# A further wait for GpSimd in the first group of a feed-forward stage, on one Trainium2 core

## The reference

```
x = attention(r, k, v, w, u)            # 4 x 768 tokens, 8 heads of 48: 3072 x 384
h = x @ w_in                            # 384 -> 2048
g = h - tanh(h)
x2 = g @ w_out                          # 2048 -> 384
e = argmax(normalised(x2) @ normalised(expert_emb).T / tau)
out = gate * (relu(x2 @ w1[e]) @ w2[e]) # 384 -> 1024 -> 384
```

## Time and profile before

| what | value |
|---|---|
| median of 3 runs | 871.93 us (870.47 to 874.06) |
| the profiled execution | 876.53 us, its span 874.8 us |
| busy: TensorE, VectorE, ScalarE, GpSimd | 845.3, 566.1, 482.6, 283.6 us |
| mean granted clock of TensorE | 0.981 of full speed |
| first group, masked copy of step 0 to that of step 15 | 128.93 to 199.58 us |

### The profile page before, as it was taken

The page is one execution under the profiler, slowest core; times in us unless marked ns, Lnnn a source line. Parts: engine busy times, 40 slices in busy tenths (PEclk is TensorE's granted clock), DMA queues, the critical chain, the costliest instruction groups (busy, mean ns, idle before and its releaser), DMA issues. The chain is left out here.

```text
span 874.8 us, 19145 instructions
## 1 busy us (share of the span) xinstructions
PE 845.3 (97%) x5568; PEld 742.6 (85%) x5569; DVE 566.1 (65%) x887; ACT 482.6 (55%) x1074; POOL 283.6 (32%) x321
## 2 busy tenths in 40 slices
PE   7999989999999999999999999999999999999995
PEld 6767758788998998998998998889899899989984
DVE  7979949999999999999999997512111211111120
ACT  4657766568777777877867866033332332333231
POOL 4434525323333433433343332212222232222211
PEclk8989999999999999999999999799999999999998
DMA  8999942215877877877877887298876576611100
GB/s 210 294 271 257 261 145 80 73 55 173 287 230 248 283 241 234 287 241 227 307 227 237 272 308 226 80 344 313 313 277 212 202 250 218 226 33 48 42 2 1
DMA packets 99370, 180.01 MB, mean 206 GB/s; under 512 B 10219, under 2 KB 25725, under 8 KB 99328
## 3 DMA queue, kind: packets, MB, share of 16 engines
q1 hardware_dynamic: 92000, 163.87, 57.8%
q0 software_dynamic: 3968, 10.82, 3.7%
q10 hardware_dynamic: 3360, 4.79, 1.7%
HBM read 114.96 MB, written 65.86 MB: 207 GB/s over the span
## 5 line engine op out<-in xcount | busy, mean ns | idle before, releaser
L1162 POOL TENSOR_TENSOR ew_l<-ew_raw,ew_h 128x512 fp32r<-128x512 f32 x96 | 126.5, 1325 | 215.0 <-DVE poly L1380 210.7
L1077 PE MATMUL y_ps<-wout_h,g_h 128*128 128x392 f32 x384 | 132.0, 344 | 3.0 <-ACT x_sb L1281 2.6
L1078 PE MATMUL y_ps<-wout_l,g_h 128*128 128x392 f32 x384 | 130.5, 340 | 0.0
L1079 PE MATMUL y_ps<-wout_h,g_l 128*128 128x392 f32 x384 | 130.4, 340 | 0.0
L1534 DVE TENSOR_TENSOR ex_hT_l<-e_bank,ex_hT_h 128x512 fp32r<-128x512 f32 x62 | 40.0, 686 | 125.3 <-ACT ex_hT_h L1690 125.3
L1077 PE MATMUL h_ps<-xT_h,win 128*128 (+1 forms) x288 | 114.4, 397 | 5.9 <-DVE diff L1361 5.0
L1079 PE MATMUL h_ps<-xT_h,win 128*128 (+1 forms) x288 | 113.9, 395 | 0.0
L1078 PE MATMUL h_ps<-xT_l,win 128*128 (+1 forms) x288 | 113.3, 393 | 0.0
L1261 ACT ACTIVATE g_h<-poly 128x512 fp32r<-128x512 f32 x96 | 61.0, 636 | 86.8 <-DVE poly L1380 86.1
L1690 ACT ACTIVATE ex_hT_h<-e_bank 128x512 fp32r<-128x512 f32 x62 | 33.8, 597 | 120.2 <-PE e_bank L1604 116.2
L1569 POOL DMA_INDIRECT out_dram<-ex_o_sb,put_i x31 | 31.1, 1002 | 205.2 <-ACT ex_o_sb L1674 205.2
(11 more groups left out here) (188 smaller groups left out, 1842.1 us busy)
## 6 DMA issues: line engine op xcount, KB each, us to landing
ew_raw<-in_w SPq DMA_DIRECT2D x96, 256.0 KB, 3.5
w_h<-ew_h SPq DMA_DIRECT2D x96, 256.0 KB, 3.6
w_l<-ew_l SPq DMA_DIRECT2D x96, 256.0 KB, 2.9
w_ex<-w_h SPq DMA_DIRECT2D x14, 1536.0 KB, 11.5
w_ex<-w_l SPq DMA_DIRECT2D x14, 1536.0 KB, 15.4
kv_sb<-in_kv SPq DMA_DIRECT2D x24, 384.0 KB, 7.4
krT_sb<-in_krT SPq DMA_DIRECT2D x40, 192.0 KB, 7.2
x_dram<-xt_sb ACTq DMA_DIRECT2D x48, 96.0 KB, 5.7
```

The costliest lines, as they stand in the source:

```text
L1077: pe.matmul(out, lh, rh, start=start, stop=False)
L1078: pe.matmul(out, lh, rl, start=False, stop=False)
L1079: return pe.matmul(out, ll, rh, start=False, stop=stop)
L1162: pool.tensor_tensor(ew_l[:, slot, :], raw, ew_h[:, slot, :].bitcast(F32), ALU.subtract).then_inc(ew_l_made, 1)
```

## The change

In `group` of GpSimd's program the condition `not is_first(g)` goes away, so that group 0 waits for `g_done` too, once a step, before the step's first piece. Everything else is as it was; on every engine the instructions stand in the order in which they stood.

```diff
                     for f in range(KF):
                         if last and f == KF - 1:
                             pool.wait_ge(gl_done, KF * CH)
-                        elif not is_first(g):
+                        else:
                             wait_apart(pool, passed_pool, (g_done, KF * g + f + 1))
                         for j in pieces_at(g, last, f):
                             low(g, j)
```

## The result

The changed kernel takes 861.63 us (median of 4 runs, 861.34 to 865.28) against 872.65 us before (median of 4). The ratio on record is 0.9886, with a 95% interval of 0.9851 to 0.992; it is not the plain quotient of the two medians, which is 0.9874. The same kernel in a second series took 864.75 us against 872.5, with a ratio of 0.9925 (0.9897 to 0.9953). It is faster, by about 1%; how much of the 11 us of the first series belongs to the change is what the experiments had to settle. The steps with one piece came out as long as forecast and those with two 0.18 us shorter, and VectorE gained 8.3 us where 6.83 were forecast.

The account below looks back on a forecast made before the run. VectorE was taken to bound steps 1 to 8 of the first group, about level with TensorE in the rest. Gains 0.64 + 4.75 + 1.44 = 6.83 us off 871.93 gave 865.1 us, range 861.8 to 869.0.

Parts of the forecast that it names:

- The start: First group, VectorE's line 1376 before the first masked copy: that copy comes 0.64 us earlier.
- Single pieces: First group from step 8, one GpSimd piece a step: four g_l shorter by 0.36 us each, 1.44 us less.
- Pairs: First group, eight intervals with two GpSimd pieces a step: 40.19 us becomes 35.44, 4.75 us less.
- 1.12 + 1.99 + 1.32: Two-piece interval of 4.43 us: masked copy to GpSimd's start, the pair's length, the pair's end to the next copy.
- the profiled run's 4.6 us: Whole kernel: the profiled execution lies 4.6 us above the median, and this difference was taken to carry over.
- What was costed at nothing: Behind the new wait: SyncE's raw-slot refills, TensorE's reads of win's low halves, the second group's stores; all cost nothing.
- The spare time at the gate of the second group: TensorE's products of the second group into y_ps: TensorE gets there in time by 1.3 to 3 us.
- TensorE as the bound: TensorE takes over as the bound, or GpSimd starts later: 867 us (866 to 869); chance 0.18.
- Nothing comes of it: VectorE's long operations have another cause, or later group boundaries give the time back: 871.9 us; chance 0.12.
- VectorE never shut out: Two-piece steps: g_l goes ahead of GpSimd's second piece, interval 3.88 us, about 862 us in all; chance 0.05.
- Slower by the raw slots: First group's ring of low part, refill, high part: with landings of 9.0 us the time is 876; chance 0.03.

Follow-up runs that it names:

- e6: Kernel before, with 16 identity products on TensorE ahead of step 3 of the first group; 874.94 us, feed-forward stage 418.51 against 418.53 us.
- e5: Kernel before, with GpSimd filling each first-group low part with zeros by three memsets instead of the subtraction; 858.88 us, feed-forward stage 407.59 us.
- e7: Changed kernel, but in steps 0 to 7 of the first group GpSimd waits for VectorE's next-step diff instead of the masked copy; 866.18 us, stage 413.82.
- e1: The changed kernel run again unaltered, five rounds against the kernel before; 864.75 us against 872.5, ratio 0.9925.
- e9: Changed kernel with each group's three x_high and x_low in steps 7, 11, 13 instead of 9, 11, 13; 860.37 us, ratio 0.9871.
- e10: Changed kernel with each group's three x_high and x_low in steps 3, 7, 11 instead of 9, 11, 13; 862.38 us, ratio 0.9902.
- e2: Changed kernel with the first group's new wait kept only in steps 0 to 7, those with two pieces; 865.75 us, ratio 0.9932.
- e3: Changed kernel with the first group's new wait kept only in steps 8 to 15, those with one piece; 869.95 us, ratio 0.9974.
- e8: Changed kernel with each group's three x_high and x_low in steps 7, 11, 15 instead of 9, 11, 13; 886.02 us, ratio 1.0164.

## Why the prediction was right, and where it was off

**The mechanism** was right in each part that a run could test: VectorE set the pace of the first group (e6), the two engines shut each other out an instruction at a time (e5, e7), and VectorE's gain passes TensorE whole (8.27 us on VectorE, 8.22 in the stage).

**The terms.** The start: 0.64 forecast; from the stage's start to the first copy it is 6.78 us before and 6.14 after, 0.64. Single pieces: 1.44 forecast, 30.46 - 29.01 = 1.45 measured. Pairs: 4.75 forecast, 6.18 measured. This is the term that was mis-sized. The step that was off is "1.12 + 1.99 + 1.32": the pair takes 2.02 (143.70 to 145.72) and the rest 1.32 (to 147.04), but GpSimd starts 0.92 and not 1.12 us after the copy. The intervals are therefore 4.25 us and not 4.43, and eight times 0.18 is the missing 1.4 us. I took the 1.12 from the second group as "from the same place in the loop", but the code there differs in two ways. The first group is written out, with waits on constants, where groups 1 to 4 are a loop whose waits compare with registers; and from group 1 on `low` has a second `wait_apart`, with one more wait and one more increment. The last group is written out too and has the second `wait_apart`. Its steps, VectorE and then GpSimd:

```profile
487.70 0.75 DVE L1380 COPY_PREDICATED poly<-large,diff 128x512 f32<-128x512 uint8 x1 [0.17 <-DVE poly L1376]
```

```profile
488.75 1.30 POOL L1162 TENSOR_TENSOR ew_l<-ew_raw,ew_h 128x512 fp32r<-128x512 f32 x1 [2.58 <-DVE poly L1380]
```

There GpSimd starts 1.05 us after the copy. So the loop goes with 0.06 us of the difference and what stands in `low` with the other 0.13; no experiment changed either by itself.

**The whole.** Forecast 865.1 in 861.8 to 869.0. The stage's 8.22 us off the 872.5 of the second series would be 864.3; measured were 861.63 in the first series, 0.2 under my lower end, and 864.75 in the second. To carry the profiled run's 4.6 us over was harmless, since it only led back to the median less 6.83; but the range allowed too little for how runs of one kernel differ, by about 7 us with the granted clock in e1 (861.82 to 868.9, and 868.71 to 875.32). The 0.981 of the profiled run is lower than in any of the 24 runs of before in the second series. The first series came 2.8 us below what the stage explains, and four runs don't settle why; the likeliest reading is such a draw. That the second series' 864.75 us lies so near the forecast 865.1 is luck too: the fair test is the stage, with 8.22 us against 6.83.

**What was costed at nothing** did cost nothing. ScalarE keeps 1.22 us of idle a step (1.4 forecast) and never waits for `ew_raw`. TensorE's one wait for a half of `win` is the 0.34 us on a weight load, under the 0.4 forecast. The spare time at the gate of the second group is 0.87 us, less than the 1.3 to 3 forecast: the wait ended 1.4 us earlier than forecast, as VectorE had gained more.

**The rivals.** TensorE as the bound: not here, but it is near, and e9, e10 and e5 meet it at 407 to 407.6 us. Nothing comes of it: out by e2 and e3. VectorE never shut out: e7 shows what a later start really does, one piece further on the piece waits and then shuts out line 1376; my 3.88 us for that case ignored the operation behind `g_l`. Slower by the raw slots: landings stay at 4.3 us or less, and ScalarE never waits for `ew_raw`.

## What to carry to other kernels

Put GpSimd's two-input operations beside those of VectorE that read PSUM, and count how long that stretch is: here a piece that fits cost nothing, one that reached over its end cost 0.36 us at `g_l`, and a second one 0.8 us more at line 1376. A wait that places the pieces can pay although it makes the waiting engine later. Before moving work to a step with room, look up how far the engine that needs its result runs ahead: in e8 TensorE stood 4.87 us at the first group's end for it, and the stage grew by 20 us.

## What was not expected of the hardware

- GpSimd's subtraction started 0.92 us after the start of VectorE's masked copy in the first group, mostly 1.10 to 1.12 us (up to 1.21) in groups 1 to 4, and 1.05 us in the last.
- When both engines have work that collides, they take turns. A piece of 128x384 that waited for `g_l` was 1.45 to 1.52 us long and one that met an `x_low` 1.25 to 1.29, instead of 1.01 to 1.03; each of VectorE's operations behind a piece ended 0.54 to 0.56 us after it.
- Time outside the stage moved by up to 4.5 us in attention (119.01 us in e1, 123.47 in e8) and by 2.3 us in routing (21.56 to 23.87), all of kernels whose code there is the same.
